# An attention step reordered: rows copied and stored one step later, transposes of r and k ahead of those of x, gate scores last

## What is computed

```python
for t in range(S):                      # attention
    cur = u * kt (x) vt                 # outer product per head
    y[:, :, t] = rt @ (state + cur)
    state = w * state + kt (x) vt
x = y as rows [B*S, 384]
goes = x @ w_skip > 0                   # first mixture of experts
e = argmax(x @ w_gate); gate = softmax(x @ w_gate)[e]
x[goes] += gate * (relu(x @ w1[e]) @ w2[e])
h = x @ w_in                            # dense block
out = (h * clip(h + 3, 0, 6) / 6) @ w_out
```

## Time and profile before

| | us |
|---|---|
| median of 3 runs | 728.77 |
| lowest, highest | 728.46, 728.89 |
| the profiled execution, its own time | 729.95 |
| its span, first to last instruction | 728.2 |
| attention, A(1) to the end of step 23 | 17.0 to 151.5 |
| TensorE busy | 700.8 (96%) |
| VectorE, ScalarE, GpSimd busy | 385.2, 324.0, 139.0 |

### The profile page before, as it was taken

One profiled execution on the slowest core, in us unless ns is written; L12 is line 12 of the kernel. 1 busy time (PEld: TensorE's weight loads), 2 busy tenths in 40 slices (PEclk: granted clock), 3 DMA queues, 4 the chain that ended last, 5 costly groups with the idle time before them and its releaser, 6 DMA issues.

```text
span 728.2 us, 13686 instructions
## 1 busy us (share of the span) xinstructions
PE 700.8 (96%) x5116; PEld 639.3 (88%) x5116; DVE 385.2 (53%) x771; ACT 324.0 (44%) x699; POOL 139.0 (19%) x189
## 2 busy tenths in 40 slices
PE   7999999848999999999999999999999999999998
PEld 5888888747999999989998999899999899998987
DVE  6676667474788888856543333433333333333332
ACT  4676666624565555554443332333333233323322
POOL 8746865431222222110000000000000000000000
PEclk9999999956999999999999999999999999999999
DMA  9897867113966566810002000200200020001001
GB/s 156 162 203 167 186 144 156 46 33 119 348 236 213 206 214 218 287 61 0 1 1 88 1 0 1 87 0 1 80 8 0 1 87 1 0 1 45 0 1 43
DMA packets 107017, 65.57 MB, mean 90 GB/s; under 512 B 79970, under 2 KB 102788, under 8 KB 106960
## 3 DMA queue, kind: packets, MB, share of 16 engines
q1 hardware_dynamic: 102896, 60.18, 30.8%
q0 software_dynamic: 2816, 4.60, 1.9%
q10 hardware_dynamic: 1248, 0.02, 0.1%
HBM read 53.69 MB, written 12.80 MB: 91 GB/s over the span
## 4 chain that ended last, share of the span: by engine, by line
PE 91%; ACT 4%; DVE 3%; issue 2%; DMA 1%; POOL 0%; ACTq 0%; POOLq 0%; SPq 0%; DVEq 0%
PE bank_A L922 8%; PE bank_A L923 8%; PE bank_A L921 8%; PE bank_L L921 4%; PE bank_L L923 4%; PE bank_L L922 4%; PE bank_P L921 4%; PE bank_P L922 4%; PE bank_P L923 4%; PE bank_A L858 4%; PE bank_kT L922 3%; PE bank_kT L923 3%; PE bank_kT L921 3%; PE bank_YT L922 3%; PE bank_YT L923 3%; PE bank_YT L921 3%
## 5 line engine op out<-in xcount | busy, mean ns | idle before, releaser
L1349 DVE TENSOR_TENSOR g_lo<-g,g_hi 128x512 fp32r<-128x512 f32 x96 | 66.5, 693 | 67.2 <-ACT g_hi L734 67.2
L734 ACT ACTIVATE g_hi<-g 128x512 fp32r<-128x512 f32 x96 | 60.9, 634 | 73.1 <-DVE g L1347 73.1
L1347 DVE SCALAR_TENSOR_TENSOR g<-cut,bank_A 128x512 f32<-128x512 f32 x60 | 41.3, 688 | 92.7 <-ACT cut L731 92.7
L731 ACT ACTIVATE cut<-bank_A 128x512 f32<-128x512 f32 x60 | 35.9, 599 | 101.1 <-PE bank_A L923 100.6
L923 PE MATMUL bank_A<-mT_hi,wi_lo 128*128 128x512 f32 x180 | 71.0, 394 | 0.0
L922 PE MATMUL bank_A<-mT_lo,wi_hi 128*128 128x512 f32 x180 | 70.9, 394 | 0.0
L921 PE MATMUL bank_A<-mT_hi,wi_hi 128*128 128x512 f32 x180 | 70.0, 389 | 0.0
L609 ACT ACTIVATE bank_A<-ident,own 128x128 f32<-128x128 f32 x188 | 58.3, 361 | 4.1 <-DVE A_sb L1108 2.6
L1347 DVE SCALAR_TENSOR_TENSOR g<-cut,bank_kT 128x512 f32<-128x512 f32 x36 | 24.8, 688 | 66.5 <-ACT cut L731 66.5
L731 ACT ACTIVATE cut<-bank_kT 128x512 f32<-128x512 f32 x36 | 21.6, 599 | 69.8 <-PE bank_kT L923 69.8
L921 PE MATMUL bank_A<-xgT_hi,w_hi 128*128 128x256 f32 x144 | 41.7, 290 | 1.3 <-DVE xgT_lo L1290 1.3
(11 more groups left out here) (247 smaller groups left out, 1851.0 us busy)
## 6 DMA issues: line engine op xcount, KB each, us to landing
raw<-in_moe_w_dram SPq DMA_DIRECT2D x24, 512.0 KB
raw<-in_moe_w_dram SPq DMA_DIRECT2D x7, 1536.0 KB
r_in<-in_r_dram SPq DMA_DIRECT2D x24, 192.0 KB, 4.7
k_in<-in_k_dram SPq DMA_DIRECT2D x24, 192.0 KB, 4.6
v_in<-in_v_dram SPq DMA_DIRECT2D x24, 192.0 KB, 3.6
x_scratch<-y_sb SPq DMA_DIRECT2D x24, 192.0 KB, 2.2
m_in<-x_scratch SPq DMA_DIRECT2D x5, 768.0 KB, 5.6
out_dram<-o_sb SPq DMA_DIRECT2D x10, 384.0 KB, 2.8
```

The lines of the kernel that those rows point to most:

```text
L731: eng.activation(cut[f % 2][:, :], p_H[f % 3][:, :], ACT.Relu, bias=0.5, scale=1.0 / 6.0).then_inc(s_cut, 1)
L734: eng.activation(g_hi[f % 4][:, :], g[f % 2][:, :], ACT.Copy).then_inc(s_ghi, 1)
L1347: eng.scalar_tensor_tensor(g[f % 2][:, :], cut[f % 2][:, :], 1.0, p_H[f % 3][:, :], ALU.min, ALU.mult).then_inc(s_g, 1)
L1349: eng.tensor_tensor(g_lo[f % 4][:, :], g[f % 2][:, :], g_hi[f % 4][:, :].bitcast(F32), ALU.subtract).then_inc(s_glo, 1)
```

## The change

Three edits, all in the attention's steps. On TensorE the transposes of r and k for step n + 1 come right behind A(n), then the x transposes of step n - 1, then, at b = 0, the gate scores of the chunk before. On ScalarE step n copies the rows of step n - 2 in place of those of step n - 1; the last step copies both. On SyncE step n stores the rows of step n - 2 and loads v of step n + 2; the last two stores stand behind the loop.

```diff
@@ sync
-                    if n:
-                        b0, c0 = (b - 1) % B, c - (b == 0)
+                    if n > 1:
+                        b0, c0 = (n - 2) % B, (n - 2) // B
                         store(b0, c0)
                         if c0 < NC - 1:
                             load_v(b0, c0 + 1)
...
-            store(B - 1, NC - 1)
+            for b in range(B - 2, B):
+                store(b, NC - 1)
@@ scalar, step
-                if n:
+                if n > 1:
+                    rows_out((n - 2) % B, (n - 2) // B)
+                if n == NT - 1:
                     rows_out(*before_it)
                 if n < NT - 1:
                     diagonal(n + 1, 0)
@@ tensor, step
                 m.then_inc(s_A, 1)
+                if n < NT - 1:
+                    transposes((b + 1) % B, c + (b + 1) // B)
+                if n:
+                    x_transposes((b - 1) % B, c - (b == 0))
                 if b == 0 and c:
                     logits(c - 1)
-                if n:
-                    x_transposes((b - 1) % B, c - (b == 0))
-                if n < NT - 1:
-                    transposes((b + 1) % B, c + (b + 1) // B)
                 if b == 1 and c:
                     logits_back(c - 1)
```

## The result

The changed kernel takes 723.18 us, the median of four runs (722.55 to 723.86), beside 728.75 (728.46 to 728.89) for the kernel before on the same chip: a ratio of 0.993, 95% interval 0.9917 to 0.9942. The forecast was 722.6, with a range of 719.3 to 726.0. The profiled execution took 722.55 with a span of 720.8, where the one of before took 729.95 with 728.2.

A forecast was written before the change was run, and what follows sets the result against it. TensorE, busy for 91% of the run, was taken as the bound. Its 6.45 us of idle time in the attention steps, less 0.27 and 0.04 that stay, gave 6.14: 728.77 - 6.1 = 722.6 us, range 719.3 to 726.0.

The forecast's parts named there:

- The bound and the place of the gain: Attention steps: TensorE's work bounds all but two; of 6.45 us idle time 6.14 goes, over half in steps 8, 12, 16, 20.
- The new chain: Attention step, from A through A_sb and the diagonals to the next A: 1.20 + 3.83 = 5.03 us.
- The new wait of the x transposes at cost 0: TensorE: x transposes wait for the row copy of step n - 2, covered by A and eight transposes; slack 0.7 us.
- TensorE's work taken as unchanged: TensorE's edit in the attention steps: the same instructions in another order, 0 us of work.
- the 0.29 of steps 11, 15 and 19: TensorE's idle time in each of these steps, 5.41 long with 5.12 of work; claimed to go entirely.
- a possible cost on kT: Late signal falling on k's transposes, at most 3.83 after A: bounds 0 and, in step 20, 0.2 us; taken as 0.
- The rival of another late signal: kT signalled later than bounded, by 1 us; steps 8, 12, 16, 20 lose about 2.5 together: 725.1 us, chance 0.06.
- The change doesn't do what it says: Steps 8 to 20: signal late for all TensorE's readers; 4.6 us idle stay, 1.5 won: 727.3 us, chance 0.07.
- A second hold on VectorE: Another VectorE instruction held by a GpSimd operation, at most 1.0 us in each of four chunks: 726.6 us, chance 0.04.
- The later load of v: SyncE's load for step n + 2; landing times over 8 us would stop TensorE, at 9 us 742.6 us; chance 0.04.
- the rival in which the clock stays up: Step 23: with idle time gone TensorE's clock stays at the higher level, 3.1 us more won: 719.5 us, chance 0.09.
- a different step 23: Sign in the changed profile: a step 23 unlike before, or step 8 over 6.5 us, would make the prediction wrong.

The follow-up runs named there:

- order and rows experiments: TensorE's new order alone against the kernel before: 734.25 us, 1.0159; ScalarE's and SyncE's edits alone, TensorE's old order: 722.79 us, 0.9997, on another chip 723.12 us.

## Why the prediction came out right, and where it was off

**The bound and the place of the gain: right.** TensorE's idle time inside the steps was what a reordering could win. Of the 6.45, 5.34 went, and 0.53 more came out of its busy time, which makes the 5.87. The plain steps are at 5.05, the gate-score step 12 at 6.06 and step 20 at 5.61, each equal to its work. The order and rows experiments show that both edits are needed on a chip without late signals; on one with them, where the forecast was measured, that is argued and not shown. One reading was wrong and cost nothing: the b = 2 steps have no idle time, but they are 5.43 to 5.48 long and not 5.21.

**The new chain: right to 0.02.** 1.20 + 3.83 = 5.03 was read from step 0 and step 3. Step 21, the only one with less work than that, is 5.05 (5.03 on the two chips looked at later).

**The new wait of the x transposes at cost 0: right, and its cover named rightly.** With the cover gone it costs about 0.25 in the b = 1 steps and 0.2 in the b = 2 steps behind them.

**TensorE's work taken as unchanged: off by little, to the good.** Busy time fell from 5.12 to 5.05 in plain steps and from 6.13 to 6.06 in gate-score steps, with the same instructions. The prediction took 0 for this, and the first two lines of the table above gave 1.08 for 0.45. Ends of matmuls are modelled, and no row shows where the 0.07 went; that a group waiting for a semaphore counted as busy is a guess.

**The late signal: the term that was mis-sized.** The prediction let the 0.29 of steps 11, 15 and 19 go entirely and put a possible cost on kT, bounded at 0 to 0.2 in step 20 and taken as 0. Step 20's kT was not late, but step 15's was: it starts 3.36 after A in place of 3.19, within the prediction's bound of 3.83, and costs 0.12 because step 15 has little work to hide it. More of it comes from a place that the prediction didn't look at: the second scatter now meets A itself. Timeline of step 11 of the changed kernel:

```profile
70.73 1.16 PE L861 MATMUL bank_A<-rT,kT 64*128 64x128 f32 x16
71.00 1.02 POOL L490 DMA_INDIRECT slot_scratch<-pairs,slots  x1 [4.71 <-DVEq L1199]
...
72.33 0.97 POOL L490 DMA_INDIRECT slot_scratch<-pairs,slots  x1 [0.30 <-issue]
72.34 1.29 DVE L1111 TENSOR_TENSOR A_sb<-bank_A,upto 128x512 f32<-128x512 f32 x2 [0.80 <-PE bank_A L861]
...
73.12 1.25 ACT L610 ACTIVATE bank_A<-ident,own 128x128 f32<-128x128 f32 x4 [1.30 <-DVE A_sb L1111]
...
76.17 1.16 PE L861 MATMUL bank_A<-rT,kT 64*128 64x128 f32 x16 [0.33 <-ACT bank_A L610]
```

A_sb starts 1.61 after A, in an undisturbed step 1.20. That is 0.41 late, at the moment of the second scatter's start, and 5.03 + 0.41 = 5.44 is the step's length. In step 12 A_sb is later still, 1.72 after A, and it costs nothing, because that step has 6.06 of work. So of the 0.88 of steps 11, 15 and 19 only 0.25 came. The rival of another late signal had the right mechanism mostly at the wrong tile, and the wrong price: 0.4 in steps 11 and 15, not 2.5 in the gate-score steps. Step 19 is no part of it: it is 5.31 long also on the chip without late signals and in the changed kernel without scatters, its first diagonal starting 2.27 after A in place of 2.00; the cause stays open.

Steps 8 and 16 are longer than step 12 by 0.22 and 0.35, and have 6.06 on the chip without late signals. The gate scores of step 12 and of step 16:

```profile
78.72 1.08 PE L828 MATMUL bank_L<-xT,gate_w 128*32 128x128 f32 x32
```

```profile
100.61 1.43 PE L828 MATMUL bank_L<-xT,gate_w 128*32 128x128 f32 x32
```

The whole 0.35 lies inside these 32 products, among which the program has no wait, and GpSimd's second scatter ran from 100.14 to 101.11. In step 8 the products behind them start 0.20 late. So here TensorE itself was held, which a late signal alone does not explain.

**"The change doesn't do what it says" (727.3): refuted.** The row copy was what carried the late signal into the round. Taken out, it cost step 20 nothing more (5.61, and 5.60 on the chip without the delay).

**"A second hold on VectorE" (726.6): did not come, but it is real.** In the changed kernel the copy takes 0.17, 0.17, 0.71, 0.79, 0.54 and 0.16 in the six chunks. With one scatter behind each GpSimd step, a shift of GpSimd's list by one operation, it took 2.3. My bound, at most one GpSimd operation of 1.0, was too low: it can be two. The Trainium skill, "SBUF — State Buffer", section on who interferes with whom, says that the two engines lock each other out for a whole instruction. The trace agrees with that in kind (0.98 beside an operation of 1.00), and goes further with 2.29 beside two of 1.01; why the copy wasn't let in between the two isn't shown.

**The later load of v (742.6): refuted.** v_in has no wait in the changed kernel, and its loads landed in these times, with a longest as in the earlier trace rows:

```profile
DMA to landing us min/median/max: 2.9/3.3/5.2
```

**The clock: one trace was read as the kernel's.** Step 23 ran at the lower level in the trace of before; in the changed kernel it ran at the higher one, the clock falling only behind it. The state products in step 23 of the changed kernel (ns, min/median/max, where the earlier trace rows has a mean of 424), and a window of the fall:

```profile
L882 PE MATMUL bank_YT<-rT,state x16: 269/269/320, 140.5 to 141.4; 64*64 64x128 f32 x16
```

```profile
145.50:146.00 0.50, 0.50 (x6) 0.50 (x6) 0.43 (x4) 0.00 (x0) 0.00 (x0) 0.82 0.00 0
```

The prediction had named a different step 23 as a sign that it was wrong, and by itself this looks like the rival in which the clock stays up. But the sign was badly chosen. The kernel before, unchanged, had its fall at 144.2 in one execution, at 151.4 in another and at 146.6 in a third, and the changed one at 145.8, 145.9 and 137.7. With late signals step 23 takes 6.28 in the kernel before and 6.30 in the changed one, where the fall comes behind it. Where it comes at the step's start, it takes 7.65 in either kernel, with late signals or without. So of the 7.4 between the two profiled spans 5.87 are steps and 1.35 are step 23's clock; the medians differ by 5.57.

**What the number hides.** The predicted 722.6 and the measured 723.18 are right for a chip that shows late signals. From A(1) to A(23) the kernel before takes 126.86 us with late signals and 122.0 without, the changed one 120.99 and 119.8. So the delay made 4.9 us of the attention before and makes 1.2 now; the change takes away 3.7 of it, and 2.2 besides. On a chip without the delay only the 2.2 are there. Step 23 holds another 1.8 of the delay in both kernels, where its clock is high, and neither the sum nor the change touches it. I said that I couldn't name the cause, and yet priced its removal as certain; a rival for it, "the delay isn't there on another chip, and 2 us are won", belonged in the list.

## What to carry to other kernels

When a copy waits in its own step for work that stands late in another engine's list, taking it from a step earlier removes it from the round; but its buffer's release then makes a new wait on the other engine, and something of the copy's length has to stand ahead of that wait, or the gain is lost there. Read the new round's length from a step that lacks the copy (here step 0), and compare it with the busy time of each kind of step before you sum. A delay whose cause the trace doesn't show should be looked for in a second execution on another chip before it is counted as won. The same holds for a clock level read from one trace.

## What the runs showed of the hardware

- **Signals of TensorE reach ScalarE and VectorE late beside two or more indirect DMAs of GpSimd in a row, on some chips.** The same kernel took 728.0 to 731.1 us on three occasions and 722.4 on two. The delay was up to 1.07 us beside two scatters and 1.8 beside four (A_sb 3.03 after A in place of 1.21), and it struck what TensorE was signalling then: mostly the x transposes before, A after. In step 8 TensorE's own next products started on time, 3.56 after A; in step 16 of the changed kernel its 32 gate-score products took 1.43 in place of 1.08. Without scatters in the same trace the steps have their undisturbed lengths. The cause is open.
- **A VectorE copy of 128x8 took between 0.16 and 2.39 us**, by what GpSimd ran beside it: 0.16 to 0.19 in all chunks once the scatters were left out, up to 1.04 before, 2.29 to 2.39 when two GpSimd operations of 1.01 followed each other over it.
- **The granted clock's fall at the end of the attention moved between 137.7 and 151.4 us** in executions that differ by nothing or little. Executions of the changed kernel on one chip went from 719.04 at a mean granted clock of 0.988 to 723.72 at 0.981, and the latter is the one whose clock fell at 137.7.
